# GpSimd's share of the weight preparation in the first stretch of a fused scan and Strassen-Winograd feed-forward kernel, in another order

## The chip, the cores and the metric

The kernel runs on one core of one Trainium2 chip. The metric is device microseconds of one execution of the whole program, as the median of several runs. Engine names: TensorE (PE: matmuls; PEld: its weight loads), VectorE (DVE), ScalarE (ACT), GpSimd (POOL), SyncE (SP: issues the DMAs).

## What is computed

A gated recurrence over time, then a feed-forward block on its states:

```python
sig = 1 / (1 + exp(-f_logit))                      # (2, 6080, 256)
f   = lower_bound + (1 - lower_bound) * sig
h_t = f_t * h_(t-1) + (1 - f_t) * x_t              # per channel, over 6080 steps
u   = h @ w_in                                     # 256 -> 2048
g   = u * clip(u + 3, 0, 6) / 6
y   = g @ w_out                                    # 2048 -> 256
```

Everything is float32. Each matmul operand is split in a rounded part (`hi`, type fp32r) and the rest (`lo` = value - `hi`), and each product is three matmuls: hi by hi, hi by lo, lo by hi.

## The kernel before, in words

Channels lie on the 128 partitions (two halves, K = 2), time along the free axis. w_in and w_out are loaded once and stay in SBUF, each as `hi` and `lo`; the raw values lie at the address of `lo` (`w7_raw` under `w7_lo`, `w_out_raw` under `w_out_lo`), so that taking the rest happens in place.

The work has two stages. The **head** (the first 960 tokens of batch 0, as 448 and 512 tokens) is done with plain products: 32 units v (2 pieces by 16 slices of 128 of the 2048 inner channels). For unit v, TensorE makes `head_up(v)` (6 matmuls into one of four PSUM banks), ScalarE `head_clip(v)` (L531), VectorE `head_gate_h(v)` (L780), ScalarE rounds (`head_round_g`, L539), VectorE takes the rest `g_lo` (`head_rest_of_g`, L786) and TensorE makes `head_down(v)` (6 matmuls, L910 to L912), which needs that rest. TensorE's queue is written as down(v - 4), up(v), down(v - 3), up(v + 1) and so on. VectorE's queue is, for each v: gate_h(v), rest of g(v - 1), and then what the list at L799 to L830 hangs on i = v - 4: the rests of w_in's blocks (`rest_of_w4`, L738), the drive, gate and scan of the head's second piece (L745, L751, L762; i from 1 to 4), and drive, gate and scan of tile 0 (L672, L678, L691; i from 12 to 19).

The **tiles** (23 of them, 1024 tokens, the first 960) use a seven-product scheme of Strassen and Winograd on w_in: w7 holds, for each of 8 blocks j, seven 128x128 matrices. Four are w_in's own, one is a difference (`make_s3`, L331), and three are the **weight sums** S1, S2, S4 (`sum_weights`, L313, L315, L318: three additions or subtractions in a chain, for a group of blocks). The groups are blocks 0-1, 2-4 and 5-7 (`GROUPS`), so that one operation is 256 or 384 elements wide. ScalarE rounds a group's sums in one cast (`round_sums(i)`, L442, 768 or 1152 wide) and GpSimd then takes their rests (`rest_of_sums(i)`, L324, as wide). TensorE needs them from the first tile on (L925). The tiles' operands (t1 to t4 and the rests `rest_of_op`, L355 to L387) are made on GpSimd, too.

Every engine has one queue, in the order in which the program lists its instructions, and semaphores tie them together; nothing plans the order but the lists in the code. GpSimd's list (L390 to L425) decides where the sums stand: all 8 rests of w_out (`rest_of_w_out(j)`, L349) and the rest of the head's operand (`rest_of_head_op`, L343) come first, then the sums of groups 0 and 1, and the rests of the sums and the sums of group 2 between the operands of tile 0. Each `rest_of_w_out(j)` waits for ScalarE's rounding (L451), which ScalarE's list has at v = 1 and at i = 1, 3, ..., 11. ScalarE's list (L555 to L602) has `round_sums` at i = 13, 15 and 19.

SP's list loads x, z, w_in and w_out first; later loads wait for the buffers of a tile to be read. No DMA is issued by GpSimd or ScalarE.

Of the kernel before, what the change touches and what calls it, by code (L numbers as in the profile page):

```python
# [29 lines left out]
def build(nc, x, z, lb, w_in, w_out, y):  # L30
# [3 lines left out]
    BLOCKS = F // 2  # L34
# [8 lines left out]
    GROUPS = (slice(0, 2), slice(2, 5), slice(5, 8))  # L43
    assert K == 2 and BLOCKS == 8 and FIRST_SPAN % (2 * RUN) == 0 and N < FIRST_SPAN <= 2 * N and STEPS >= 2

    with ExitStack() as ctx:
# [113 lines left out]
        def half_span(t):  # L160
            return FIRST_SPAN // 2 if t == 0 else N
# [9 lines left out]
        def raw_of(at):  # L171
            if at.stop <= 2:
                return h_sb[:, at].rearrange("p j (c m) -> p j c m", m=P)
            return w_in_raw[:, at.start - 2:at.stop - 2]
# [35 lines left out]
        def pair(j):  # L210
            return slice(2 * j, 2 * j + 2)
# [90 lines left out]
        def _(pool):  # L302
            def rest_of_w4(j):
                pool.wait_ge(w4_hi_ready, j + 1)
                nc.gpsimd.tensor_tensor(w7_lo[:, j, 0:4], raw_of(one_block(j))[:, 0],
                                        w7_hi[:, j, 0:4].bitcast(F32), ALU.subtract).then_inc(w4_ready[j], 1)

            def sum_weights(i):
                at = GROUPS[i]
                raw, to = raw_of(at), w7_raw[:, at]  # L310
                for j in range(at.start, at.stop):
                    pool.wait_ge(w_in_loaded[j], 16)
                nc.gpsimd.tensor_tensor(to[:, :, S1_T1], raw[:, :, 2], raw[:, :, 3], ALU.add).then_inc(w_sums_ready, 1)  # L313
                pool.wait_ge(w_sums_ready, 3 * i + 1)
                nc.gpsimd.tensor_tensor(to[:, :, S2_T2], to[:, :, S1_T1], raw[:, :, 0],  # L315
                                        ALU.subtract).then_inc(w_sums_ready, 1)
                pool.wait_ge(w_sums_ready, 3 * i + 2)
                nc.gpsimd.tensor_tensor(to[:, :, S4_B22], raw[:, :, 1], to[:, :, S2_T2],  # L318
                                        ALU.subtract).then_inc(w_sums_ready, 1)

            def rest_of_sums(i):
                at = GROUPS[i]
                pool.wait_ge(w_sums_hi_ready, i + 1)
                nc.gpsimd.tensor_tensor(w7_lo[:, at, 4:7], w7_raw[:, at, 4:7], w7_hi[:, at, 4:7].bitcast(F32),  # L324
                                        ALU.subtract).then_inc(w_sums_lo_ready, 1)
# [14 lines left out]
            def rest_of_head_op():  # L340
                at = head_tokens(1)
                pool.wait_ge(head_op_hi_ready, 3)
                nc.gpsimd.tensor_tensor(op_lo_odd[:, 2:4, 0:HEAD_N[1]], x_sb[:, :, at],  # L343
                                        op_hi_odd[:, 2:4, 0:HEAD_N[1]].bitcast(F32),
                                        ALU.subtract).then_inc(head_op_ready[2], 1)

            def rest_of_w_out(j):
                pool.wait_ge(w_out_hi_ready, j + 1)
                nc.gpsimd.tensor_tensor(w_out_lo[:, pair(j)], w_out_raw[:, pair(j)],  # L349
                                        w_out_hi[:, pair(j)].bitcast(F32), ALU.subtract).then_inc(w_out_ready, 1)  # L350

            def rest_of_op(t, o):
                n = half_span(t)
                pool.wait_ge(op_hi_ready[o], t + 1)
                nc.gpsimd.tensor_tensor(packed(operand_lo(t, o), n), source_of(o, n),  # L355
                                        packed(operand_hi(t, o), n).bitcast(F32),
                                        ALU.subtract).then_inc(op_ready[o], 1)

            def make_t1(t):
                n = half_span(t)  # L360
                pool.wait_ge(state_ready[0], 2 * (t + 1))
                if t > 0:
                    pool.wait_ge(op_ready[A22_T4], t)
                nc.gpsimd.tensor_tensor(packed(t_a, n), state_half(0, SECOND, n), state_half(0, FIRST, n),  # L364
                                        ALU.subtract).then_inc(t1_ready, 1)

            def make_t2(t):
                n = half_span(t)
                pool.wait_ge(state_ready[1], 2 * (t + 1))
                pool.wait_ge(t1_ready, t + 1)  # L370
                if t > 0:
                    pool.wait_ge(op_ready[S2_T2], t)
                nc.gpsimd.tensor_tensor(packed(t_b, n), state_half(1, SECOND, n), packed(t_a, n),
                                        ALU.subtract).then_inc(t2_ready, 1)

            def make_t3(t):
                n = half_span(t)
                if t > 0:
                    pool.wait_ge(op_ready[S3_T3], t)
                nc.gpsimd.tensor_tensor(packed(t_c, n), state_half(1, SECOND, n), state_half(0, SECOND, n),  # L380
                                        ALU.subtract).then_inc(t3_ready, 1)
# [7 lines left out]

            rest_of_w4(1)  # L390
            rest_of_w4(2)
            for j in range(5):
                rest_of_w_out(j)
            rest_of_head_op()
            for j in range(5, BLOCKS):
                rest_of_w_out(j)
            sum_weights(0)
            sum_weights(1)
            rest_of_sums(0)
            for t in range(TILES):  # L400
                make_t1(t)
                rest_of_op(t, A11_B11)
                if t == 0:
                    rest_of_sums(1)
                rest_of_op(t, S1_T1)
                if t == 0:
                    sum_weights(2)
                make_t2(t)
                rest_of_op(t, A12_B21)
                rest_of_op(t, S4_B22)  # L410
                rest_of_op(t, S2_T2)
                if t == 0:
                    rest_of_sums(2)
                make_t3(t)
                make_t4(t)
                if t == 0:
                    make_s3(0)
                rest_of_op(t, S3_T3)
                rest_of_op(t, A22_T4)
                if t == 0:  # L420
                    rest_of_s3(0)
                    make_s3(1)
                    rest_of_s3(1)
                    make_s3(2)
                    rest_of_s3(2)  # L425

        @block.scalar
        def _(act):
# [10 lines left out]
            def round_sums(i):  # L439
                at = GROUPS[i]  # L440
                act.wait_ge(w_sums_ready, 3 * (i + 1))
                nc.scalar.copy(w7_hi[:, at, 4:7], w7_raw[:, at, 4:7]).then_inc(w_sums_hi_ready, 1)  # L442
# [112 lines left out]
            for v in range(HEAD):  # L555
                head_clip(v)
                if v > 0:
                    head_round_g(v - 1)
                i = v - LEAD
                if v == 1:  # L560
                    round_w_out(1)
                if i >= 0 and i % 2 == 0 and 4 + i // 2 < BLOCKS:
                    round_w4(4 + i // 2)
                if i >= 0 and i % 2 == 1 and 2 + i // 2 < BLOCKS:
                    round_w_out(2 + i // 2)
                if i == 0:
                    head_sig(2)
                if i == 5:
                    head_round_op(2)
                if i == 9:  # L570
                    make_sig(0, 0)
                if i == 10:
                    make_sig(0, 1)
                if i == 13:
                    round_sums(0)
                if i == 15:
                    round_sums(1)
                if i == 16:
                    round_op(0, A11_B11)
                if i == 18:  # L580
                    head_copy_y(0, 0)
                    round_op(0, S1_T1)
                if i == 19:
                    head_copy_y(0, 1)
                    round_sums(2)
                if i == 20:
                    round_op(0, A12_B21)
                if i == 21:
                    round_op(0, S4_B22)
                if i == 22:  # L590
                    round_op(0, S2_T2)
                if i == 23:
                    make_sig(1, 0)
                if i == 24:
                    round_op(0, S3_T3)
                if i == 25:
                    round_op(0, A22_T4)
                if i == 26:
                    round_s3(0)
                if i == 27:  # L600
                    make_sig(1, 1)
                    round_s3(1)  # L602
            head_round_g(HEAD - 1)
            for q in range(LAST + 1):
                t, j = divmod(q, BLOCKS)
# [49 lines left out]
            t, n = TILES - 1, half_span(TILES - 1)  # L655
# [382 lines left out]
```

## Time and profile before

| | |
|---|---|
| median of 3 runs | 1006.11 us (1005.99 to 1008.08) |
| the profiled execution's own time | 1006.84 us |
| its span | 1004.8 us |
| mean granted TensorE clock over the span | 0.996 of full speed |
| busy: PE, DVE, ACT, POOL | 990.6, 823.4, 710.8, 222.0 us |

In the profile an instruction's row gives its start, its duration, engine, line, operation, output and inputs with their shape (128 partitions by so many elements). A duration includes time in which the instruction has started and is held up by something other than a semaphore. In brackets stands the time that the engine was idle ahead of it and what released it; where there is no bracket, it followed the instruction before it.

### The profile page before, as it was taken

The numbers are of one execution on the slowest core, as the hardware profiler recorded it, in microseconds if no ns is written. First come the engines' busy times: TensorE is split into PE (matmuls) and PEld (weight loads), VectorE is DVE, ScalarE is ACT, GpSimd is POOL, SyncE is SP. The second block draws the span as 40 slices with busy tenths as digits, with TensorE's granted clock in tenths as the row PEclk, the third lists the DMA queues.
The fourth block names the chain that finished last, engine by engine and source line by source line (L and its number), as shares of the span: only waits on it lengthen the run. The fifth ranks groups of instructions, "written<-read, shape, count | busy, mean of one in ns | idle before, by whom it ended". The sixth has DMA issues, their size and how long they took to land.

```text
span 1004.8 us, 12906 instructions
## 1 busy us (share of the span) xinstructions
PE 990.6 (99%) x4372; PEld 821.4 (82%) x4372; DVE 823.4 (82%) x1170; ACT 710.8 (71%) x1208; POOL 222.0 (22%) x154
## 2 busy tenths in 40 slices
PE   8999999999999999999999999999999999999997
PEld 6877888888888888888888888888888888888886
DVE  6898898887898888788788789788878878887665
ACT  5756667767767777777776777777777777677665
POOL 2488024003113111211401311311121140131000
PEclk8999999999999999999999999999999999999999
DMA  6203002102100110110110110011011011001001
GB/s 246 80 0 102 22 22 64 48 14 64 42 22 23 41 63 22 43 63 6 59 46 17 64 43 22 22 42 64 21 42 64 4 61 42 1 1 42 1 1 43
DMA packets 13522, 42.38 MB, mean 42 GB/s; under 512 B 1424, under 2 KB 2192, under 8 KB 13456
## 3 DMA queue, kind: packets, MB, share of 16 engines
q1 hardware_dynamic: 13456, 41.56, 12.2%
q8 instruction: 35, 0.57, 0.2%
q14 instruction: 31, 0.25, 0.1%
HBM read 29.10 MB, written 12.45 MB: 41 GB/s over the span
## 4 chain that ended last, share of the span: by engine, by line
PE 94%; DVE 4%; ACT 1%; issue 1%; DMA 0%; SPq 0%; DVEq 0%
PE y_ps L946 16%; PE y_ps L947 16%; PE y_ps L948 16%; PE x_ps L928 8%; PE x_ps L929 8%; PE x_ps L930 8%; PE v_ps L928 4%; PE v_ps L930 4%; PE v_ps L929 4%; PE z_ps L930 2%; PE z_ps L929 2%; PE z_ps L928 2%; PE y_ps L910 1%; PE y_ps L911 1%; PE y_ps L912 1%; DVE g_lo L786 1%
## 5 line engine op out<-in xcount | busy, mean ns | idle before, releaser
L724 DVE TENSOR_TENSOR g_lo<-g,g_hi 128x512 fp32r<-128x512 f32 (+1 forms) x352 | 271.9, 773 | 45.8 <-ACT g_hi L501 45.1
L946 PE MATMUL y_ps<-g_hi,w_out_hi 128*128 128x512 f32 (+1 forms) x704 | 274.2, 389 | 1.6 <-DVE g_lo L724 1.6
L947 PE MATMUL y_ps<-g_lo,w_out_hi 128*128 128x512 f32 (+1 forms) x704 | 273.3, 388 | 0.0
L948 PE MATMUL y_ps<-g_hi,w_out_lo 128*128 128x512 f32 (+1 forms) x704 | 273.2, 388 | 0.0
L501 ACT CAST g_hi<-g 128x512 fp32r<-128x512 f32 (+1 forms) x352 | 209.0, 620 | 16.9 <-DVE g L719 16.7
L946 PEld LDWEIGHTS y_ps<-g_hi,w_out_hi 128*128 128x128 f32 x704 | 132.1, 188 | 31.0 <-ACT y_sb L511 2.3
L948 PEld LDWEIGHTS y_ps<-g_hi,w_out_lo 128*128 128x128 f32 x704 | 132.1, 188 | 26.7
L947 PEld LDWEIGHTS y_ps<-g_lo,w_out_hi 128*128 128x128 f32 x704 | 132.2, 188 | 26.4
L492 ACT ACTIVATE g<-z_ps,half 128x512 f32<-128x512 f32 (+1 forms) x88 | 60.5, 687 | 57.6 <-DVE z_ps L702 56.4
L492 ACT ACTIVATE g<-v_ps,half 128x512 f32<-128x512 f32 (+1 forms) x88 | 60.4, 687 | 55.7 <-DVE v_ps L714 55.7
L708 DVE TENSOR_TENSOR h_sb<-v_ps,h_sb 128x512 f32<-128x512 f32 (+1 forms) x88 | 60.5, 688 | 34.7 <-PE v_ps L930 33.4
L481 ACT COPY h_sb<-x_ps 128x512 f32<-128x512 f32 (+1 forms) x88 | 51.5, 585 | 47.6 <-PE x_ps L930 47.6
L702 DVE TENSOR_TENSOR z_ps<-z_ps,h_sb 128x512 f32<-128x512 f32 (+1 forms) x88 | 61.1, 694 | 24.0 <-PE z_ps L930 24.0
L492 ACT ACTIVATE g<-h_sb,half 128x512 f32<-128x512 f32 (+1 forms) x88 | 63.6, 723 | 22.3 <-DVE h_sb L708 22.1
L928 PE MATMUL x_ps<-op_hi_even,w_hi 128*128 128x512 f32 (+1 forms) x192 | 74.6, 388 | 1.7 <-ACT h_sb L471 1.6
L471 ACT COPY h_sb<-x_ps 128x512 f32<-128x512 f32 (+1 forms) x88 | 51.3, 583 | 33.7 <-PE x_ps L930 33.7
L719 DVE SCALAR_TENSOR_TENSOR g<-g,x_ps 128x512 f32<-128x512 f32 (+1 forms) x88 | 59.7, 679 | 18.8 <-ACT g L492 18.8
L929 PE MATMUL x_ps<-op_lo_even,w_hi 128*128 128x512 f32 (+1 forms) x192 | 74.4, 387 | 0.0
L930 PE MATMUL x_ps<-op_hi_even,w_lo 128*128 128x512 f32 (+1 forms) x192 | 74.3, 387 | 0.0
L364 POOL TENSOR_TENSOR t_a<-x_sb 128x512 f32<-128x512 f32 (+1 forms) x11 | 15.0, 1362 | 265.9 <-DVE x_sb L691 265.9
L719 DVE SCALAR_TENSOR_TENSOR g<-g,v_ps 128x512 f32<-128x512 f32 (+1 forms) x88 | 60.2, 684 | 14.6 <-ACT g L492 14.6
L719 DVE SCALAR_TENSOR_TENSOR g<-g,h_sb 128x512 f32<-128x512 f32 (+1 forms) x88 | 60.4, 687 | 11.7 <-ACT g L492 11.2
(152 smaller groups left out, 1860.9 us busy)
## 6 DMA issues: line engine op xcount, KB each, us to landing
z_sb<-in_z SPq DMA_DIRECT2D x21, 512.0 KB, 3.5
x_sb<-in_x SPq DMA_DIRECT2D x21, 512.0 KB, 4.4
out_y<-y_sb SPq DMA_DIRECT2D x9, 1024.0 KB, 4.2
w_out_raw<-in_w_out SPq DMA_DIRECT2D x8, 256.0 KB, 6.9
w_in_raw<-in_w_in SPq DMA_DIRECT2D x6, 256.0 KB, 6.3
out_y<-y_sb SPq DMA_DIRECT2D x3, 512.0 KB, 2.6
z_sb<-in_z SPq DMA_DIRECT2D x2, 480.0 KB, 4.1
x_sb<-in_x SPq DMA_DIRECT2D x2, 480.0 KB, 4.2
```

What stands on the lines that cost most here:

```text
L492: nc.scalar.activation(g[:, u, 0:n], up_result(q, u, n), ACT.Relu, bias=half[:], scale=1.0 / 6.0).then_inc(clipped_ready[u], 1)
L501: nc.scalar.copy(g_hi[:, u, 0:n], g[:, u, 0:n]).then_inc(g_hi_ready[u], 1)
L702: nc.vector.tensor_tensor(z_ps[:, 0:n], z_ps[:, 0:n], h_sb[:, C11, 0:n], ALU.add).then_inc(h_ready[C11], 1)
L708: nc.vector.tensor_tensor(h_sb[:, C22, 0:n], v_ps[:, 0:n], h_sb[:, C22, 0:n], ALU.add).then_inc(h_ready[C22], 1)
L719: nc.vector.scalar_tensor_tensor(g[:, u, 0:n], g[:, u, 0:n], 1.0, up_result(q, u, n), ALU.min, ALU.mult).then_inc(g_ready[u], 1)
L724: nc.vector.tensor_tensor(g_lo[:, u, 0:n], g[:, u, 0:n], g_hi[:, u, 0:n].bitcast(F32), ALU.subtract).then_inc(g_lo_ready[u], 1)
L928: nc.tensor.matmul(out[:, 0:n], w_hi, x_hi, start=start, stop=False, skip_group_check=True)
L929: nc.tensor.matmul(out[:, 0:n], w_hi, x_lo, start=False, stop=False, skip_group_check=True)
L930: return nc.tensor.matmul(out[:, 0:n], w_lo, x_hi, start=False, stop=True, skip_group_check=True)
L946: nc.tensor.matmul(out, w_out_hi[:, f, at], g_hi[:, u, 0:n], start=opens, stop=False)
L947: nc.tensor.matmul(out, w_out_hi[:, f, at], g_lo[:, u, 0:n], start=False, stop=False)
L948: return nc.tensor.matmul(out, w_out_lo[:, f, at], g_hi[:, u, 0:n], start=False, stop=closes)
```

## The change

GpSimd makes the sums of group 0 behind the rest of w_out's pair 1, those of group 1 behind that of pair 2, and those of group 2 behind that of pair 5; the three rests of the sums stand one behind the other after the rest of pair 7, ahead of all of tile 0's operands. ScalarE rounds the sums at i = 8, 10 and 12 instead of 13, 15 and 19. Nothing is added or left out, and no DMA is touched.

```diff
             rest_of_w4(1)
             rest_of_w4(2)
-            for j in range(5):
-                rest_of_w_out(j)
+            rest_of_w_out(0)
+            rest_of_w_out(1)
+            sum_weights(0)
+            rest_of_w_out(2)
+            sum_weights(1)
+            rest_of_w_out(3)
+            rest_of_w_out(4)
             rest_of_head_op()
-            for j in range(5, BLOCKS):
-                rest_of_w_out(j)
-            sum_weights(0)
-            sum_weights(1)
-            rest_of_sums(0)
+            rest_of_w_out(5)
+            sum_weights(2)
+            rest_of_w_out(6)
+            rest_of_w_out(7)
+            for i in range(len(GROUPS)):
+                rest_of_sums(i)
             for t in range(TILES):
                 make_t1(t)
                 rest_of_op(t, A11_B11)
-                if t == 0:
-                    rest_of_sums(1)
                 rest_of_op(t, S1_T1)
-                if t == 0:
-                    sum_weights(2)
                 make_t2(t)
                 rest_of_op(t, A12_B21)
                 rest_of_op(t, S4_B22)
                 rest_of_op(t, S2_T2)
-                if t == 0:
-                    rest_of_sums(2)
                 make_t3(t)
...
-                if i == 13:
-                    round_sums(0)
-                if i == 15:
-                    round_sums(1)
+                if i in (8, 10, 12):
+                    round_sums((i - 8) // 2)
                 if i == 16:
                     round_op(0, A11_B11)
...
                 if i == 19:
                     head_copy_y(0, 1)
-                    round_sums(2)
```

## Rows read from the trace of the kernel before

**Rows 1.** The page: busy time of each engine over the span.

```profile
PE 990.6 (99%) x4372; PEld 821.4 (82%) x4372; DVE 823.4 (82%) x1170; ACT 710.8 (71%) x1208; POOL 222.0 (22%) x154
```

**Rows 2.** Busy time by stretch: PE, PEld, DVE, ACT, POOL, clock, DMA share, GB/s.

```profile
20.00:26.40 6.40, 6.32 (x32) 5.47 (x31) 5.58 (x11) 4.92 (x9) 0.21 (x2) 1.00 0.01 3
26.40:44.20 17.80, 17.80 (x87) 15.89 (x85) 17.73 (x24) 11.65 (x21) 8.55 (x5) 1.00 0.30 90
44.20:52.40 8.20, 8.16 (x40) 7.38 (x40) 4.43 (x8) 6.50 (x12) 2.70 (x2) 1.00 0.12 48
52.40:62.40 10.00, 10.00 (x48) 8.55 (x47) 9.61 (x9) 6.20 (x10) 9.30 (x8) 1.00 0.00 0
62.40:82.40 20.00, 18.06 (x76) 13.73 (x75) 19.88 (x22) 11.20 (x20) 15.06 (x9) 1.00 0.22 72
```

**Rows 3.** Timeline of PE: the head's first matmul of down(6), and the restarts after stalls.

```profile
34.23 0.37 PE L910 MATMUL y_ps<-g_hi,w_out_hi 128*128 128x448 f32 x1
...
44.33 0.44 PE L910 MATMUL y_ps<-g_hi,w_out_hi 128*128 128x448 f32 x1
...
62.37 0.39 PE L910 MATMUL y_ps<-g_hi,w_out_hi 128*128 128x512 f32 x1
...
70.30 0.39 PE L900 MATMUL v_ps<-op_hi_odd,w_lo 128*128 128x512 f32 x1
72.39 0.50 PE L910 MATMUL y_ps<-g_hi,w_out_hi 128*128 128x512 f32 x1 [1.70 <-DVE g_lo L786]
...
99.16 0.48 PE L928 MATMUL x_ps<-op_hi_even,w_hi 128*128 128x480 f32 x1 [1.58 <-ACT h_sb L471]
```

**Rows 4.** Timeline of POOL from 20 to 92 us.

```profile
26.20 1.29 POOL L349 TENSOR_TENSOR w_out_lo<-w_out_raw,w_out_hi 128x512 fp32r<-128x512 f32 x1 [6.19 <-ACT w_out_hi L451]
31.16 1.41 POOL L349 TENSOR_TENSOR w_out_lo<-w_out_raw,w_out_hi 128x512 fp32r<-128x512 f32 x1 [3.67 <-ACT w_out_hi L451]
...
38.25 2.69 POOL L343 TENSOR_TENSOR op_lo_odd<-x_sb,op_hi_odd 128x1024 fp32r<-128x1024 f32 x1
41.26 1.30 POOL L349 TENSOR_TENSOR w_out_lo<-w_out_raw,w_out_hi 128x512 fp32r<-128x512 f32 x1 [0.33 <-ACT w_out_hi L451]
...
57.01 1.35 POOL L315 TENSOR_TENSOR w_raw<-w_raw,w_in_raw 128x384 f32<-128x384 f32 x1
59.72 2.29 POOL L324 TENSOR_TENSOR w_lo<-w_raw,w_hi 128x768 fp32r<-128x768 f32 x1
...
68.22 3.57 POOL L324 TENSOR_TENSOR w_lo<-w_raw,w_hi 128x1152 fp32r<-128x1152 f32 x1
```

**Rows 5.** Timeline of DVE from 26 to 45 us.

```profile
26.25 1.78 DVE L745 SCALAR_TENSOR_TENSOR x_sb<-z_sb,one_minus_lb,x_sb 128x512 f32<-128x512 f32 x1
28.07 0.49 DVE L751 TENSOR_SCALAR z_sb<-z_sb,lb_minus_one 128x512 f32<-128x512 f32 x1
...
31.86 1.19 DVE L786 TENSOR_TENSOR g_lo<-g,g_hi 128x448 fp32r<-128x448 f32 x1
...
38.73 0.62 DVE L780 SCALAR_TENSOR_TENSOR g<-g,z_ps 128x448 f32<-128x448 f32 x1
39.27 2.15 DVE L786 TENSOR_TENSOR g_lo<-g,g_hi 128x448 fp32r<-128x448 f32 x1
41.34 1.77 DVE L738 TENSOR_TENSOR w_lo<-w_in_raw,w_hi 128x512 fp32r<-128x512 f32 x1
...
43.57 0.61 DVE L786 TENSOR_TENSOR g_lo<-g,g_hi 128x448 fp32r<-128x448 f32 x1
```

**Rows 6.** Timeline of DVE from 54 to 73 us.

```profile
56.57 0.91 DVE L786 TENSOR_TENSOR g_lo<-g,g_hi 128x512 fp32r<-128x512 f32 x1
...
69.80 2.54 DVE L786 TENSOR_TENSOR g_lo<-g,g_hi 128x512 fp32r<-128x512 f32 x1
```

**Rows 7.** Timeline of ACT: one rounding of sums, and the end of the head.

```profile
60.94 1.16 ACT L442 CAST w_hi<-w_raw 128x1152 fp32r<-128x1152 f32 x1
...
96.67 1.06 ACT L432 ACTIVATE z_sb<-z_sb 128x1024 f32<-128x1024 f32 x1
```

## The prediction, made before the changed kernel was timed

> **What bounds the kernel now.** I read the page first: PE is busy for 990.6 of 1004.8 us, VectorE for 823, GpSimd for 222 [rows 1]. So only time that TensorE loses can be won, and GpSimd's work counts by what it does to others. The busy table by stretch shows that the engines' means hide two stretches in which VectorE is full: from 26.4 to 44.2 us it is busy for 17.73 of 17.80 us, and from 52.4 to 82.4 for 29.49 of 30.00. Between them, from 44.2 to 52.4, it is busy for only 4.43 of 8.20 [rows 2]. PE's timeline gives the losses. From 62.37 to 70.30 it starts 35 matmuls, one per 0.227 us; then comes a gap of 2.09 us up to 72.39, ended by a `g_lo` of VectorE [rows 3]. The stretch from 62.4 to 82.4 holds 76 matmuls where 88 fit [rows 2]: 12 lost, at 0.227 some 2.8 us; with the rounding I put it at 2.9. Before 50 us there is one small loss, the restart at 44.33, and after the head one of 1.6 to 1.8 ahead of 99.16, where PE waits for ScalarE's copy [rows 3].
>
> **Why VectorE is full there.** I laid GpSimd's timeline beside VectorE's. When a GpSimd operation is running, a VectorE operation with two inputs in SBUF, or the gate (L751), doesn't go on until it ends. The rest of g at 39.27 took 2.15 us where an undisturbed one takes 0.61 [rows 5]; GpSimd's operation of 38.25 ended at 40.94 [rows 4], the rest at 41.42, so 0.48 behind it. The next pairs agree: GpSimd ends at 42.56 [rows 4], VectorE's L738 at 43.11 [rows 5]. It holds the other way, too: GpSimd's 1.35 us at 57.01 [rows 4] begin under a rest that ends at 57.48 [rows 6], so 0.88 us are its own. The two take turns, one operation each. An operation that reads PSUM isn't held: `gate_h` at 38.73 took 0.62 under the same GpSimd operation [rows 5]. GpSimd's own time by width comes out as 0.65 (256), 0.88 (384), 1.15 (512: 41.42 to 42.56), 2.3 (1024) and, for the rests of the sums, 1.70 (768: 60.31 to 62.01) and 2.51 (1152: 69.28 to 71.79) [rows 4]; 0.65, 60.31 and 69.28 are ends of VectorE's neighbouring operations, read in the same way. The Trainium skill says as much (GPSIMD Engine Reference, section 8, Key points): GpSimd shares its SBUF interfaces with VectorE and contends with VectorE instructions that have two SBUF inputs or run in a 2-port mode. By the rows and that rule the moved work costs what follows; if idle time on GpSimd were free, the sum would be only the gain of 2.9 us, which is the first rival.
>
> **What is moved.** No operation is added or dropped. The nine operations of `sum_weights` (2.0 + 2.6 + 2.6 us of GpSimd's own time) go from behind 52.4 us into 20 to 48; the three rests (1.7 + 2.5 + 2.5) end up in one run behind the last rest of w_out; ScalarE's three casts (0.8 to 1.16 us [rows 7]) come at i = 8, 10, 12. No DMA and no entry of SP's queue moves; the loads of tile 0 that wait for the head's operand come later by what the head loses, and have some 8 us to spare.
>
> **Step 1, sums of group 0: 0.1 us.** They fall into 20 to 23.5, where VectorE has 0.8 us idle (5.58 busy of 6.40 [rows 2]). They delay one rest of g that PE waits for anyway, by 0.1. All later times below hold this 0.1.
>
> **Step 2, sums of group 1: 2.3 us.** They follow the rest of pair 2, which starts at 26.20 and ends at 27.49 [rows 4]. VectorE's order from there is: drive (26.25), gate (28.07), gate_h 6, rest 5, L738, drive, gate, gate_h 7, rest 6 (31.86) [rows 5]. With turns taken: the first sum runs from 28.13 to 29.01 and holds the gate, +0.65 beside the 0.1; the second waits for the gate, runs under gate_h 6 and holds rest 5 until 30.19, +0.30; the third holds L738 until 31.55, +0.82; the rest of pair 3 (31.16 [rows 4], its rounding no later) then holds the second drive instead of rest 6, +1.03 there and -0.58 on rest 6. Rest 6 ended at 33.05 [rows 5] and now ends at 33.05 + 0.1 + 0.65 + 0.30 + 0.82 + 1.03 - 0.58 = 35.37. PE wants it for down(6) at 34.23 + 0.1 [rows 3]: a stall of 1.1 where there was none. VectorE has no idle time up to 44.2, so rests 8 and 9 keep the 2.32 us: 41.42 becomes 43.74.
>
> **Step 3, first sum of group 2: 0.3 us.** It comes between the rest of pair 5 and rest 10, which started at 43.57 [rows 5]: it runs partly under a gate_h and adds 0.42 less the 0.13 of start-up that a held operation has behind it. Rest 10 ends 2.6 us later than at 44.18, and since PE's restart at 44.33 followed it directly [rows 3], PE is **2.6 us** behind from there. The other two sums lie in VectorE's idle 3.8 us (44.2 to 52.4 [rows 2]) and cost nothing; if that cover were gone, they would cost up to 1.8. Bounds of the first loss: 2.0 (VectorE wins two turns) and 3.3 (each sum held in full).
>
> **Step 4, the three rests in one run.** Times here are those of before, so without the 2.6. ScalarE's cast of group 1 (1.16) stands in one round with a sigmoid of 1.0 and puts the rounding of w_out's last pair 1 us later; GpSimd is done with it at 53.4. There rest 15 and the rest of the group 0 sums ask at the same time. If VectorE is first: rest of sums 0 to 55.6, drive to 56.6, rest of sums 1 to 59.1, rest 16 at 59.65 just in time, rest of sums 2 to 62.16, which holds the gate of tile 0, and rest 17 comes at 63.8 where PE wants it at 62.37 [rows 3]: 1.4 us lost, then 0.2 to 0.4 at rest 20, as VectorE is full. That is 1.8. If GpSimd is first, rest 16 comes at 62.25 where 59.65 is wanted: 2.6 to 2.8. I take 1.9, near the first, because VectorE's operation is released in the earlier step of the two. Bounds: 1.2 (VectorE's backlog alone, if all gate_h lie under a hold) and 2.8.
>
> **Step 5, what goes.** The rest of sums 1 that held rest 20 until 71.79 (69.80 + 2.54 [rows 6], 68.22 + 3.57 [rows 4]) is gone from there, and the sums of group 2 behind it: the 2.9 us of 70 to 82 go. By my turns rests 19 to 23 have 0.4 to 1.2 us to spare after step 4. The wait ahead of 99.16 [rows 3] stays: ScalarE does there the last clip, a rounding, a sigmoid of 1.06 (96.67 [rows 7]), the cast of a difference and a rounding, and GpSimd being early shortens none of it.
>
> **Sum.** +2.6 + 1.9 - 2.9 = +1.6 us. Made against the profiled execution it gives 1006.84 + 1.6; the median of the runs shown is 0.7 lower, so the median after should be 1006.11 + 1.6 = **1007.7 us**.
>
> **The rivals.** (A) GpSimd's gaps are free: the sums fit into waits of 3.7 and 6.2 us [rows 4] and VectorE makes good what it is held up. Then only step 5 counts: 1006.1 - 2.9 = 1003.2 us. For it: ScalarE has idle time and PE runs four units ahead. Against it: VectorE's 17.73 of 17.80. (B) The second run of rests is hidden, the first loss is not: 2.6 - 2.9, 1005.8 us. For it: PE's lead is larger after its stalls. Against it: 29.49 of 30.00. (C) Slower by more than a measurement can tell: at the tie of step 4 GpSimd gets the first turn, its three rests are all ahead of rest 16, and the second loss is 2.8 instead of 1.9: 1006.1 + 2.6 + 2.8 - 2.9 = 1008.6 us. It decides if the last rest of w_out ends before rest 15 is released, 0.05 us apart by my count, so it is near to even. (D) The change does nothing, because the sums wait for something else: their inputs were loaded by 20 us (DMA share 0.01 from 20 to 26.4 [rows 2]), so I give it nothing.
>
> **Numbers.** Forecast 0.42 (1007.0 to 1008.1), C 0.33, B 0.12, A 0.13. About 0.2%, 2.0 us, is what a measurement of this kernel can tell from no change. Faster: A, 0.13. Slower: C and the upper edge of the forecast, 0.35. The same: 0.52. The range leaves A out and takes in B and C with the bounds of steps 2 to 4: 1005.2 to 1009.3.
>
> **What would show it.** In the changed profile: sums of group 1 between 27 and 32 us with durations above 1.2 each; VectorE without idle time from 26 to 47; PE waiting for `g_lo` L786 near 34 to 47 us for some 2.5 us in all, and again near 62 to 67 for 1.4 to 2.8; no gap of 2 us at 70 to 82; the wait for ScalarE's copy at the end of the head still there. I would be wrong if VectorE's operations with two SBUF inputs were not held under the moved sums, if PE had no stall before 50 us, or if the second stall were missing.

## The result, and the profile after

The change makes the kernel slower by a quarter of a per cent: 1009.38 us (median of 7, 1007.68 to 1010.96) beside 1006.03 us of the kernel before (median of 7), ratio 1.0026 (95% interval 1.0016 to 1.0035). A second row of runs on another occasion gave the same: 1009.29 us beside 1006.24 us, ratio 1.0030 (1.0019 to 1.0040). The loss is 2.6 and 3.0 us by these ratios and 3.4 and 3.1 us by the medians, and both intervals leave out "no change". So the gain that one would expect from work moved into idle time of GpSimd did not come.

The page first, with the rows that answer to [rows 1]. Columns as there.

```profile
span 1007.3 us, 12906 instructions
PE 990.7 (98%) x4372; PEld 821.4 (82%) x4372; DVE 819.3 (81%) x1170; ACT 710.6 (71%) x1208; POOL 221.1 (22%) x154
```

The span is 2.5 us longer, no engine has more work, and VectorE is even busy for 4.1 us less. (Time in which a VectorE operation is held up counts as busy, and in total there is less of it than before.) PE's busy time is the same, so the page's sums don't show where the 2.5 us went. The busy table by stretch can (PE, PEld, DVE, ACT, POOL, clock, DMA share, GB/s; it answers to [rows 2]):

```profile
10.00:20.00 10.00, 7.96 (x30) 5.97 (x30) 7.47 (x9) 5.89 (x12) 5.50 (x5) 0.83 1.01 386
26.40:47.00 20.60, 18.62 (x88) 15.89 (x88) 20.53 (x26) 12.96 (x24) 14.83 (x11) 1.00 0.30 96
55.00:65.00 10.00, 8.04 (x36) 6.49 (x35) 10.00 (x8) 4.35 (x7) 7.92 (x3) 1.00 0.00 0
65.00:68.40 3.40, 3.40 (x10) 2.61 (x9) 3.40 (x5) 0.97 (x3) 0.00 (x0) 0.51 0.00 0
```

From 26.4 to 47 us PE now has 2 us without work where it had next to none (20.56 of 20.60 us busy before), and VectorE is full (20.53 of 20.60). From 55 to 65 us it is full again and PE lacks another 2 us. And from 65 to 68.4 us the granted clock is 0.51: TensorE runs at its lower level of 1.2 GHz, which the kernel before showed only ahead of 20 us.

PE's timeline at these places (answers to [rows 3]):

```profile
33.06 0.37 PE L897 MATMUL x_ps<-op_hi_odd,w_lo 128*128 128x448 f32 x1
34.47 0.44 PE L907 MATMUL y_ps<-g_hi,w_out_hi 128*128 128x448 f32 x1 [1.04 <-DVE g_lo L783]
...
40.07 0.44 PE L907 MATMUL y_ps<-g_hi,w_out_hi 128*128 128x448 f32 x1 [0.52 <-DVE g_lo L783]
...
45.87 0.44 PE L907 MATMUL y_ps<-g_hi,w_out_hi 128*128 128x448 f32 x1 [0.39 <-DVE g_lo L783]
...
61.16 0.40 PE L897 MATMUL v_ps<-op_hi_odd,w_lo 128*128 128x512 f32 x1
63.52 0.50 PE L907 MATMUL y_ps<-g_hi,w_out_hi 128*128 128x512 f32 x1 [1.96 <-DVE g_lo L783]
...
66.25 0.63 PE L895 MATMUL x_ps<-op_hi_odd,w_hi 128*128 128x512 f32 x1
66.67 0.63 PE L896 MATMUL x_ps<-op_lo_odd,w_hi 128*128 128x512 f32 x1
```

Every restart behind a wait is released by a rest of g; the last two rows are not waits but the half clock. The starts are 0.21 us (448 columns) or 0.227 us (512 columns) apart where PE runs freely; what is beyond that is the loss. Added up over the head, against the kernel before (us):

| place | before | after | difference |
|---|---|---|---|
| first 24 us (loads, low clock, sums of group 0) | | | -1.0 |
| 24 to 50 us, waits for rests of g | 0.3 | 2.9 | +2.6 |
| near 61 us, wait for rest 16 | 0 | 2.2 | +2.2 |
| 65 to 68.4 us, half clock: 8 starts 0.427 apart instead of 0.227 | 0 | 1.6 | +1.6 |
| 70 to 82 us, waits for rests of g | 2.9 | 0 | -2.9 |
| end of the head, wait for ScalarE | 1.8 | 1.8 | 0 |

The sum is +2.5 us, and so much the spans differ. Without the first line it is +3.5 us, of which the waits are 1.9 and the clock is 1.6.

The first line can't be put down to the change. PE starts the first matmul of down(2) at 23.34 us here and at 24.31 in the kernel before, and the granted clock from 10 to 20 us is 0.83 here and 0.66 there. But this time varies without any change: in the second profile of the changed kernel it is 24.07 us, with the same 0.83, and in the three profiles of one kernel at the end of the experiments 23.18, 23.88 and 24.49. So the 1.0 us is no more than single executions differ by, and how much of it is the low clock stays open.

### The profile page after: what moved, and what is told of

Read it like the earlier page. It is cut to its first block, busy times and chain, and to the rows that moved or that the text cites. A ratio compares the mean times of both kernels' runs of the same rounds, so it can differ in the third digit from the quotient of the medians.

```text
span 1007.3 us, 12906 instructions
## 1 busy us (share of the span) xinstructions
PE 990.7 (98%) x4372; PEld 821.4 (82%) x4372; DVE 819.3 (81%) x1170; ACT 710.6 (71%) x1208; POOL 221.1 (22%) x154
## 4 chain that ended last, share of the span: by engine, by line
PE 92%; DVE 5%; ACT 1%; issue 1%; DMA 0%; SPq 0%; DVEq 0%; ACTq 0%
PE y_ps L943 16%; PE y_ps L944 16%; PE y_ps L945 16%; PE x_ps L925 8%; PE x_ps L926 8%; PE x_ps L927 8%; PE v_ps L925 4%; PE v_ps L927 4%; PE v_ps L926 4%; PE z_ps L927 2%; PE z_ps L925 2%; PE z_ps L926 2%; DVE g_lo L783 1%; PE y_ps L907 1%; PE y_ps L908 1%; PE y_ps L909 1%
```

## The experiments

A "stall" or a "loss" below is what lies beyond the usual spacing of PE's starts; a "gap" is the whole time from one start to the next. Each kernel was timed beside the kernel before on the same chip, but not all on one chip; the kernel before had medians of 1006.24 to 1006.53 us on them.

**The changed kernel again, for its spread.**

> The changed kernel as it is, for a row of runs beside the other three. Theory of the clock (the stall of 2.4 us near 61, gap of 2.36 us between two matmuls, makes the chip halve TensorE's clock for one stretch of 3.4 us in most runs, at 1.6 us each): two groups of runs again, at 1007.7 and at 1009.4, most in the upper one. Rival (the upper group comes from the first 20 us, where loads and the clock vary from run to run): the spread is like that of the kernel before, 1.5 us, with no second group.

Measured: 1009.29 us (7 runs, 1008.01 to 1010.77). The profiled execution has the same stalls (3.1 us before 50 us, a gap of 2.48 us near 62) and again 3.4 us at half clock right behind the gap. Two groups of runs can't be told apart, so this decides nothing between the theory and the rival: ahead of 24 us alone the two profiles of this kernel differ by 0.7 us. The mean granted clock is 0.9959 in both rows of seven runs, beside 0.9971 in the 23 runs of the kernel before on this chip and 0.9974 in 28 on another. One stretch of 3.4 us at half clock in 1007 us is 0.0017. The difference of 0.0012 to 0.0015 therefore suggests that most executions have one such stretch more than before; only two of them were looked at.

**Sums of groups 1 and 2 where VectorE has idle time.**

```diff
             rest_of_w_out(2)
-            sum_weights(1)
             rest_of_w_out(3)
             rest_of_w_out(4)
             rest_of_head_op()
             rest_of_w_out(5)
-            sum_weights(2)
+            sum_weights(1)
             rest_of_w_out(6)
+            sum_weights(2)
             rest_of_w_out(7)
```

> Edit to the changed kernel: the sums of group 1 move from behind the rest of pair 2 to behind the rest of pair 5, those of group 2 behind the rest of pair 6; all else as changed. Theory (GpSimd and VectorE take turns, and only work put where VectorE has no idle time costs): the stalls of 34 to 46 us fall from 2.8 us to 0.3 to 0.6, the stall of 2.1 us near 61 stays, so 2.2 us less than the changed kernel in a run with an equal clock: 1005.5 us without a drop of the clock, 1007.1 with one. Rival 1 (the loss comes from the rests of w_out being late, TensorE waiting for w_out and not for g's rest): the sums ahead of pair 6 and 7 delay those as much, and the time stays at 1007.7 to 1009.4. Rival 2 (only the drop of the clock costs): no difference from the changed kernel.

Measured: 1007.22 us (11 runs, 1005.44 to 1008.77), ratio to before 1.0007 (0.9999 to 1.0016). The six sums are the same, 5.3 us of GpSimd's own time; only their place is another. PE now has work for 20.12 of 20.60 us between 26.4 and 47.

```profile
26.40:47.00 20.60, 20.12 (x99) 17.96 (x98) 19.73 (x28) 15.03 (x27) 13.30 (x8) 1.00 0.30 96
...
55.00:65.00 10.00, 7.72 (x28) 6.07 (x27) 10.00 (x9) 2.51 (x4) 5.52 (x2) 0.83 0.00 0
```

99 matmuls instead of 88 fit there. The loss before 50 us is 0.9 instead of 2.9, of it 0.6 at rest 10, which the first sum of group 1 holds: a little more than the 0.3 to 0.6 expected. The stall near 61 is still there (gap 2.66 us), and so is the half clock behind it (0.83 over 55 to 65 us). The median is the 1007.1 that was expected with a drop of the clock. Three of the 11 runs lie at 1005.4 to 1005.9 us, near the 1005.5 expected without one, two of them at a mean clock of 0.998; no such run was profiled. Rivals 1 and 2 both had the loss before 50 us stay; it fell by 2.0 us, so both fall.

**The rests of the sums where they were.**

```diff
-            for i in range(len(GROUPS)):
-                rest_of_sums(i)
+            rest_of_sums(0)
...
                 rest_of_op(t, A11_B11)
+                if t == 0:
+                    rest_of_sums(1)
                 rest_of_op(t, S1_T1)
...
                 rest_of_op(t, S2_T2)
+                if t == 0:
+                    rest_of_sums(2)
                 make_t3(t)
```

> Edit to the changed kernel: the rests of the sums of groups 1 and 2 go back to their places before the change (between the operands of tile 0). Theory: the stalls of 34 to 46 us stay at 2.8 us, the stall near 61 is gone since only the 1.7 us rest of group 0 is held there, and the rest of group 1 near 70 meets a VectorE with no backlog, so at most 0.3 us is lost there; the clock doesn't drop. About as before the change: 1006.0 us (1005.6 to 1006.6). Rival 1 (any place of these rests costs VectorE the same 2.5 us each): 1007.7. Rival 2 (only the drop of the clock costs): 1006.0 minus what the three rests cost before, 1003 to 1004, with no stall before 50 us worth naming.

Measured: 1006.24 us (11 runs, 1004.71 to 1007.37), ratio 0.9997 (0.9988 to 1.0006). PE loses 3.0 us before 50 us (restarts at 35.70, 41.31, 44.07 and 47.11), and nothing from 50 us to the end of the head; the clock stays full there. So this kernel has the first loss of the changed kernel, 2.7 us more than before, and lacks the 2.9 us that the kernel before loses at 70 to 82 us; the two nearly cancel.

**One of the three rests later.**

```diff
-            for i in range(len(GROUPS)):
-                rest_of_sums(i)
+            rest_of_sums(0)
+            rest_of_sums(1)
...
                 rest_of_op(t, A11_B11)
+                if t == 0:
+                    rest_of_sums(2)
                 rest_of_op(t, S1_T1)
```

> Edit to the changed kernel: only the rest of the sums of group 2 moves behind the rest of tile 0's first operand. Theory: rest 16 of g comes 2.5 us earlier, the stall near 61 falls from 2.1 to under 0.4 us, up to 0.6 us is lost near 68 to 72, the clock doesn't drop in any run since there is no gap over 1.4 us ahead of the one at the end of the head: 1006.5 us (1006.0 to 1007.2). Rival (the drop of the clock doesn't hang on that stall): runs of about 1.6 us more still appear, as often as with the changed kernel (5 of 7).

Measured: 1008.16 us (11 runs, 1007.23 to 1008.54), ratio 1.0016 (1.0007 to 1.0025): outside what was expected. The stall near 61 fell to 0.5 us (under 0.4 was expected), but the moved rest met a rest of g in turn, and 1.4 us were lost near 74 instead of at most 0.6:

```profile
70.77 3.59 POOL L324 TENSOR_TENSOR w_lo<-w_raw,w_hi 128x1152 fp32r<-128x1152 f32 x1
```

```profile
69.66 2.17 DVE L671 SCALAR_TENSOR_TENSOR x_sb<-z_sb,one_minus_lb,x_sb 128x960 f32<-128x960 f32 x1
...
72.35 2.56 DVE L785 TENSOR_TENSOR g_lo<-g,g_hi 128x512 fp32r<-128x512 f32 x1
```

GpSimd's 3.59 us contain the end of VectorE's drive (to 71.83) and then 2.5 us of its own (to 74.36); the rest of g starts at 72.35 and ends at 74.91, 0.55 behind it. The mean clock is 0.997 or 0.998 in each of the 11 runs (the changed kernel has 0.994 to 0.998), and the profiled one has no half clock after 20 us. So nothing in these runs shows a halving once the long gap is gone, as the theory said.

**Both edits.** The first two diffs together.

> Both edits at once: sums of groups 1 and 2 behind the rests of pairs 5 and 6, rests of the sums of groups 1 and 2 where they were before the change. Theory: no loss over 0.6 us before 50 us, none near 61, at most 0.3 near 70: 2.2 to 2.6 us below before the change, 1003.6 us. Rival (VectorE pays for GpSimd's own time wherever it stands): 1006.

Measured: 1003.46 us (6 runs, 1003.01 to 1004.13), ratio 0.9971 (0.9959 to 0.9982). It beats both kernels, by 2.8 us the one before. Between 24 us and the wait at the end of the head PE loses 0.9 us, of it 0.6 at rest 10.

**ScalarE's roundings later, so that VectorE gets the first turn.**

```diff
-                if i in (8, 10, 12):
-                    round_sums((i - 8) // 2)
+                if i in (12, 13, 14):
+                    round_sums(i - 12)
```

> Edit to the changed kernel: ScalarE rounds the sums at i = 12, 13 and 14 instead of 8, 10 and 12, so that GpSimd's three rests can't begin before rest 15 of g is released. Theory (at the tie of step 4 the order of turns decides): rest 15 and the drive of tile 0 go first, the stall near 61 falls from 2.1 us to 0.2 to 1.3 us, and the clock isn't halved: 1006.9 us (1006.3 to 1007.7), 1.0 to 2.5 below the changed kernel. The losses before 50 us stay at 2.8. Rival (only the sum of GpSimd's time counts, not the order): the stall stays above 2 us, 1009 us.

Measured: 1007.61 us (11 runs, 1007.09 to 1009.25), ratio 1.0014 (1.0005 to 1.0022). Inside the expected range. Rest 15 and the drive went first, as the rows of VectorE show:

```profile
54.91 0.62 DVE L783 TENSOR_TENSOR g_lo<-g,g_hi 128x448 fp32r<-128x448 f32 x1
55.44 1.21 DVE L669 SCALAR_TENSOR_TENSOR x_sb<-z_sb,one_minus_lb,x_sb 128x960 f32<-128x960 f32 x1
...
57.50 1.42 DVE L783 TENSOR_TENSOR g_lo<-g,g_hi 128x512 fp32r<-128x512 f32 x1
58.84 3.14 DVE L675 TENSOR_SCALAR z_sb<-z_sb,lb_minus_one 128x960 f32<-128x960 f32 x1
...
62.50 2.56 DVE L783 TENSOR_TENSOR g_lo<-g,g_hi 128x512 fp32r<-128x512 f32 x1
```

The stall is one rest later (rest 17, 1.3 us, at 65.12) and is followed by 0.4 us near 73.7: 1.7 in all instead of 2.2, and no halving in this profile. So the order of turns is worth 0.5 us of waits. The medians differ by 1.7 us; the rest of that fits the halving that is gone with the shorter gap, but that was seen in this one profile only.

**The end of the head.**

```diff
                 if i == 27:
-                    make_sig(1, 1)
                     round_s3(1)
...
+                if q == 1:
+                    make_sig(1, 1)
                 if j == 4 and beyond:
```

> Edit to the kernel with both edits (1003.5 us): the sigmoid of the second half of tile 1, 1.06 us of ScalarE at the end of the head, moves into block 1 of tile 0. Theory (the gap of 1.98 us at the end of the head is ScalarE's own chain of work ahead of its first copy, as step 5 says, and GpSimd has no part in it): the gap falls by 1.0 us to about 1.0, total 1002.5 us. Rival (the copy waits for GpSimd's difference ahead of it on ScalarE's queue): no change, 1003.5.

Measured: 1002.79 us (5 runs, 1002.16 to 1004.00), ratio 0.9963 (0.9950 to 0.9977). That is 0.7 us below the kernel with both edits, where 1.0 was expected. The gap at the end of the head is 1.03 us instead of 1.98, as expected, so it is ScalarE's own work that PE waits for there and the rival falls:

```profile
95.15 0.49 PE L929 MATMUL x_ps<-op_hi_even,w_hi 128*128 128x480 f32 x1 [0.64 <-ACT h_sb L474]
```

**The sums one pair later still.** On top of the last one: sums of group 1 behind pair 6, of group 2 behind pair 7, roundings at i = 8, 11, 15.

> Edit to the kernel of b2_sigmoid_later: sums of group 1 behind the rest of pair 6 and those of group 2 behind that of pair 7, ScalarE's roundings at i = 8, 11, 15. Theory: the last loss of 0.5 us at 43 us goes, because the first sum of group 1 no longer holds rest 10 of g, and the later sums meet a VectorE with 2.4 us in hand at 52 us: 0.5 us less than b2, 1002.0 us, if that reserve holds; 0.5 us more than b2 if it doesn't, with a new stall between 60 and 72 us.

Measured: 1005.02 us (11 runs, 1003.62 to 1005.64), ratio 0.9984 (0.9975 to 0.9993). The loss at 43 us went, as expected (0.3 us are left before 50 us instead of 0.9). But the reserve did not hold: PE loses 1.2 us near 72, and the wait at the end of the head is 0.7 us longer than in the last kernel. The time is outside both values expected (1002.0 and 1003.3). Of the 2.3 us between the two profiled executions, 0.7 lie ahead of 24 us and may be spread.

**Is the half clock a matter of the gap?** The rests of groups 1 and 2 as one instruction, on top of both edits:

```diff
+            def rest_of_two_groups():
+                at = slice(2, 8)
+                pool.wait_ge(w_sums_hi_ready, 3)
+                nc.gpsimd.tensor_tensor(w7_lo[:, at, 4:7], w7_raw[:, at, 4:7], w7_hi[:, at, 4:7].bitcast(F32),
+                                        ALU.subtract).then_inc(w_sums_lo_ready, 2)
...
                 if t == 0:
-                    rest_of_sums(1)
+                    rest_of_two_groups()
...
-                if t == 0:
-                    rest_of_sums(2)
```

> Edit to the kernel with both edits (1003.5 us, no stall between 50 and 90 us, clock full after 24 us): the rests of the sums of groups 1 and 2 are one GpSimd instruction of 2304 elements at the place of the first, instead of two of 1152. By the rows of the other kernels it runs for some 5.0 us alone, so that rest 20 of g is held 2.5 us longer. Theory (a gap of over 2.3 us between two matmuls, wherever it stands, is followed by a stretch of 3.4 us at half clock, one of up to 2.1 isn't): a gap of 2.4 to 2.9 us between 67 and 71 us, the clock at half for 3.4 us behind it, 1003.5 + 2.4 + 1.6 = 1007.5 us (1006.8 to 1008.2). Rival (the halving belongs to something else near 61 to 65 us, where it was seen three times): the gap alone, 1005.9 us, the clock at full speed.

Measured: 1005.64 us (11 runs, 1005.34 to 1007.41), ratio 0.9996 (0.9987 to 1.0005). The gap came out at 2.23 us, shorter than aimed at, with the clock full behind it. That tells the two apart badly, so all three groups were put into one instruction (`at = slice(0, 8)`, the rest of group 0 taken out of its place):

> As c1_one_wide_rest, but the rests of all three groups are one instruction of 3072 elements at the place of group 1's (6.7 us by itself), since c1's gap of 2.23 us lay below the smallest gap that a halving followed (2.36). Theory (a longer gap anywhere here is followed by 3.4 us at half clock): a gap of 3.3 to 3.9 us near 68 to 73 us, half clock behind it, 1003.5 + 3.4 + 1.6 = 1008.5 us (1007.9 to 1009.2). Rival (the halving belongs to something else near 61 to 65 us): the gap alone, clock full, 1006.9 us.

Measured: 1008.86 us (11 runs, 1007.33 to 1010.77), ratio 1.0024 (1.0015 to 1.0033). The median fits the theory. The profiled execution (1007.33) does not: it has a gap of 3.83 us, as expected, and the full clock behind it. VectorE's row is the clearest of all for the turns, a rest of 0.68 us that takes 6.64:

```profile
65.27 7.67 POOL L330 TENSOR_TENSOR w_lo<-w_raw,w_hi 128x3072 fp32r<-128x3072 f32 x1
```

```profile
66.84 6.64 DVE L789 TENSOR_TENSOR g_lo<-g,g_hi 128x512 fp32r<-128x512 f32 x1
```

The 11 runs lie at 1007.3 (three), 1008.4 to 1009.0 (five) and 1010.4 to 1010.8 (three). So the same kernel was looked at twice more.

> The kernel of c2_wider_rest once more, one execution with a profile. Its 11 runs lie in groups near 1007.3, 1008.8 and 1010.6 us, and its profiled one (1007.3, gap of 3.83 us) kept the full clock behind the gap. Theory (whether the clock is halved behind a gap hangs on where the gap falls in time, not on its length alone): with a time near 1008.8 or 1010.6 the profile shows 3.4 us or more at half clock right behind the gap, with one near 1007.3 it shows none. Rival (the groups come from the first 20 us): a time of 1008.8 or more without a halving behind the gap.

> As c2_look2, a third execution of the same kernel with a profile: by the counts of the 11 runs it has a chance of 2 in 3 to fall into one of the upper groups, and then shows the half clock behind the gap by the theory, and not there but ahead of 20 us by the rival.

Measured: 1009.29 and 1010.21 us. Both have the gap of 3.84 us and 3.4 us at half clock behind it. The stretches of the first look, then of the second, then of the third:

```profile
10.00:20.00 10.00, 7.96 (x31) 6.01 (x30) 7.50 (x9) 6.21 (x12) 5.51 (x5) 0.83 1.01 387
70.00:80.00 10.00, 6.56 (x29) 5.26 (x29) 10.00 (x9) 3.20 (x6) 4.77 (x3) 1.00 0.20 61
```

```profile
10.00:20.00 10.00, 8.55 (x29) 6.94 (x29) 7.13 (x10) 5.57 (x11) 5.17 (x4) 0.72 1.00 384
70.00:75.00 5.00, 1.54 (x6) 0.99 (x5) 5.00 (x2) 0.93 (x2) 5.00 (x2) 0.87 0.00 0
75.00:80.00 5.00, 5.00 (x19) 4.04 (x18) 5.00 (x7) 2.25 (x4) 0.26 (x1) 0.79 0.25 87
```

```profile
10.00:20.00 10.00, 8.21 (x26) 6.34 (x25) 6.53 (x7) 5.38 (x11) 4.62 (x4) 0.66 1.03 387
75.00:80.00 5.00, 5.00 (x16) 3.96 (x17) 5.00 (x7) 1.56 (x3) 0.86 (x1) 0.66 0.13 49
```

The halving costs 1.6 us in the third look, as in the changed kernel, and 1.3 us in the second: there it begins some 0.5 us before PE restarts at 74.25, so that part of it falls into the gap. It follows the gap wherever that stands, so it isn't tied to anything else near 61 us; but one and the same gap is followed by it in two executions and not in a third. The other difference between the three lies ahead of 24 us, where the second is 0.7 and the third 1.3 us behind the first. The granted clock differs there, too (0.83, 0.72 and 0.66 from 10 to 20 us).

## Why the prediction was right, and where it was short

Forecast was a loss of 1.6 us, 1007.7 us. Measured was a loss of 2.6 to 3.0 us by the ratios (1.6 to 4.0 by their intervals) and of 3.1 to 3.4 by the medians. On 1006.11 us the ratios make 1008.7 and 1009.1, near the upper edge of the range (1009.3); the first median, 1009.38, lies just above it. The turns of the two engines, on which every step rests, came out row by row. The likeliest case fell short in two terms: the order of turns at step 4, and the clock, which had no term at all. That the range still held the result was in part luck: its upper edge was made of the bounds of steps 2 to 4, and 1.6 us of the loss come from something else.

- **Turns of GpSimd and VectorE.** Shown, by rows and by runs: the same sums go with 2.9 us of lost PE time when those of group 1 stand at 26 to 31 us and those of group 2 at 43 to 48, and with 0.9 when they stand at 41 to 46 and 47 to 51 us, at the end of VectorE's full stretch and behind it. The Trainium skill (SBUF — State Buffer, Who interferes with whom) states this as contention for a shared port pair, which it calls an exclusive lock, between a GpSimd instruction that reads SBUF and a VectorE instruction with two SBUF inputs. The trace agrees, and here the lock lasts for the whole instruction: 6.64 us for a rest of 0.68 under one GpSimd instruction. The rival that GpSimd's gaps are free (A) gave the sign wrong.
- **Step 1**, 0.1 us: PE has no stall at 20 to 24 us in the changed kernel; whether it is 0.1 us later can't be read, since single executions differ by up to 1.3 us there.
- **Steps 2 and 3**, 2.6 us: measured +2.6 (2.9 less 0.3). The first stall was foretold at 1.1 us for down(6) and is 1.2. The turns are those of the forecast. GpSimd and VectorE in the changed kernel:

```profile
26.48 1.48 POOL L313 TENSOR_TENSOR w_raw<-w_in_raw 128x384 f32<-128x384 f32 x1
28.04 1.08 POOL L315 TENSOR_TENSOR w_raw<-w_raw,w_in_raw 128x384 f32<-128x384 f32 x1
29.20 1.28 POOL L318 TENSOR_TENSOR w_raw<-w_in_raw,w_raw 128x384 f32<-128x384 f32 x1
30.44 1.75 POOL L349 TENSOR_TENSOR w_out_lo<-w_out_raw,w_out_hi 128x512 fp32r<-128x512 f32 x1
```

```profile
27.11 1.13 DVE L748 TENSOR_SCALAR z_sb<-z_sb,lb_minus_one 128x512 f32<-128x512 f32 x1
...
28.69 0.91 DVE L783 TENSOR_TENSOR g_lo<-g,g_hi 128x448 fp32r<-128x448 f32 x1
29.52 1.50 DVE L735 TENSOR_TENSOR w_lo<-w_in_raw,w_hi 128x512 fp32r<-128x512 f32 x1
30.95 1.78 DVE L742 SCALAR_TENSOR_TENSOR x_sb<-z_sb,one_minus_lb,x_sb 128x512 f32<-128x512 f32 x1
```

  The last three of them in the kernel before:

```profile
29.00 0.62 DVE L786 TENSOR_TENSOR g_lo<-g,g_hi 128x448 fp32r<-128x448 f32 x1
29.54 0.69 DVE L738 TENSOR_TENSOR w_lo<-w_in_raw,w_hi 128x512 fp32r<-128x512 f32 x1
30.14 0.75 DVE L745 SCALAR_TENSOR_TENSOR x_sb<-z_sb,one_minus_lb,x_sb 128x512 f32<-128x512 f32 x1
```

  The gate grows by 0.64 us (0.65 foretold), rest 5 by 0.29 (0.30), the rest of w_in's block by 0.81 (0.82) and the second drive by 1.03 (1.03).
- **Step 4**, 1.9 us: measured 2.2. The step put ScalarE's rounding of the last pair 1 us later, and so made the tie at rest 15 go to VectorE. It was late by only some 0.5: GpSimd began its run of rests at 54.50 and rest 15 of g was released at 55.06, so that GpSimd had the first turn and all three of its rests lay ahead of the end of rest 16. GpSimd's three rests, as one row, and the rows of VectorE:

```profile
54.50 8.42 POOL L324 TENSOR_TENSOR w_lo<-w_raw,w_hi 128x768 fp32r<-128x768 f32 x3
```

```profile
55.06 1.78 DVE L783 TENSOR_TENSOR g_lo<-g,g_hi 128x448 fp32r<-128x448 f32 x1
56.77 3.64 DVE L669 SCALAR_TENSOR_TENSOR x_sb<-z_sb,one_minus_lb,x_sb 128x960 f32<-128x960 f32 x1
60.33 0.67 DVE L777 SCALAR_TENSOR_TENSOR g<-g,x_ps 128x512 f32<-128x512 f32 x1
60.92 2.54 DVE L783 TENSOR_TENSOR g_lo<-g,g_hi 128x512 fp32r<-128x512 f32 x1
```

  Three operations in turn are held by one rest each, and only the `gate_h` between them (0.67), which reads PSUM, isn't. That is rival C in its place and order, with 2.2 us where it said 2.8: GpSimd's start half a microsecond earlier put part of the first rest under a `gate_h`. With the tie turned round (ScalarE's roundings later) the loss was 1.7, beside the 1.8 that the forecast had for that order.
- **The missing term**: the clock. No step and no rival asked what the chip does behind a gap of PE. The kernel before has a gap of 2.09 us with the full clock behind it [rows 3]. The changed kernel's gap is 0.3 to 0.4 us longer, and both of its profiles have 3.4 us at 1.2 GHz behind it, which cost some 1.6 us each. The forecast with this term and with 2.2 us for step 4 would be 1006.1 + 3.5 = 1009.6 us, beside medians of 1009.38 and 1009.29. The lowest runs (1007.68 and 1007.78 us) lie where a kernel without the halving would, but none of them was profiled.
- **Step 5**, -2.9 us: right. No wait of PE at 70 to 82 us, and the wait at the end of the head is as long as before; that it is ScalarE's own was shown by moving one sigmoid, which halved the gap.

It is open what decides whether a gap is followed by the half clock. Gaps from 2.36 to 3.84 us were followed by it in five of six profiles, gaps of up to 2.23 us after the first 24 us in none. It is also open why the kernel with the sums one pair later waits 0.7 us longer at the end of the head.

## What to carry to other kernels

An engine at 22% can be the one that costs: when two engines take turns, as GpSimd and VectorE do here, moving work of the idle one into its own gaps helps only where the other one has gaps too, so look for stretches in which the **other** engine is full, and put the work outside them. Long operations of GpSimd are best kept apart from each other, so that what VectorE owes to TensorE is never behind two of them in a row. A longer gap of TensorE (2.36 us and more here) may cost another 1.3 to 1.6 us in clock, and not in every execution, so judge such a change by many runs.

## What was unexpected of the hardware

The halving of TensorE's clock in the middle of a kernel at 98% busy, behind a single gap of 2.36, 2.48 and 2.66 us, each time for 3.4 us; and that a gap of 3.83 us left the clock alone in one execution, while the same gap (3.84 us) did not in two others. Apart from that, the first 24 us alone differ by up to 1.3 us between executions of one kernel, as much as several of the edits here are worth.
